# Attention with two feed-forward blocks: the pair's sums in twos behind a slot, one low part put after a slot at the turn, and fewer waits written for TensorE

## The reference

```python
# q, k, v: (2, 8, 768, 64), n_sink 4, window 128
keep = is_sink | in_window
a = softmax(where(keep, scale * q @ k.T, -1e9)); x = a @ v          # (1536, 512)
x = (silu(x @ w_gate) * (x @ w_val)) @ w_out                        # d_ff 1536, stage B
h = x @ w_in; x = (maximum(h, 0) + alpha * minimum(h, 0)) @ w_out2  # d_ff 2048, stage C
```

## Time and profile before

| | |
|---|---|
| time, median of 3 runs | 640.73 us (639.49 to 641.68) |
| the profiled execution's own time | 638.97 us |
| its span | 637.2 us |
| TensorE matmuls busy | 622.4 us, 98% |
| TensorE weight loads busy | 488.4 us, 77% |
| GpSimd busy | 452.2 us, 71% |
| VectorE busy | 407.0 us, 64% |
| ScalarE busy | 243.8 us, 38% |
| granted TensorE clock | full in all 40 slices |

### The profile page before, as it was taken

The page is one execution under the profiler, slowest core; times in us unless marked ns, Lnnn a source line. Parts: engine busy times, 40 slices in busy tenths (PEclk is TensorE's granted clock), DMA queues, the critical chain, the costliest instruction groups (busy, mean ns, idle before and its releaser), DMA issues.

```text
span 637.2 us, 9474 instructions
## 1 busy us (share of the span) xinstructions
PE 622.4 (98%) x3072; PEld 488.4 (77%) x3072; DVE 407.0 (64%) x696; ACT 243.8 (38%) x585; POOL 452.2 (71%) x600
## 2 busy tenths in 40 slices
PE   8889999999998999999999999999999999999998
PEld 5467776777776888888888878887788888888886
DVE  5954667666475866565646474799686567756474
ACT  4735553545534642121212121435544324442150
POOL 6848778878784798999989764779999887810000
PEclk9999999999999999999999999999999999999999
DMA  9343423311321110112212222100222222000004
GB/s 299 110 150 107 136 95 112 117 51 58 97 92 37 33 34 33 67 61 72 68 33 67 89 77 66 33 19 16 67 67 66 67 66 84 17 0 1 1 15 183
DMA packets 29391, 45.67 MB, mean 72 GB/s; under 512 B 2880, under 2 KB 9024, under 8 KB 29344
## 3 DMA queue, kind: packets, MB, share of 16 engines
q1 hardware_dynamic: 29200, 44.81, 21.6%
q10 hardware_dynamic: 144, 0.26, 0.1%
HBM read 41.92 MB, written 3.15 MB: 71 GB/s over the span
## 4 chain that ended last, share of the span: by engine, by line
PE 79%; POOL 9%; DVE 5%; issue 4%; ACT 2%; DMA 1%; SPq 0%; POOLq 0%; DVEq 0%; ACTq 0%
PE ffn_ps L1972 25%; PE att_ps L1946 23%; PE ffn_ps L1887 10%; PE att_ps L1972 7%; PE ffn_ps L1946 6%; POOL w_lo L1657 2%; PE att_ps L1834 2%; POOL scratch L1737 1%; DVE scratch L2199 1%; DMA raw_weights<-pieces 1%; POOL w_hi L1656 1%; PE att_ps L1979 1%; POOL w_lo L1685 1%; PE att_ps L1796 1%; PE att_ps L1887 1%
## 5 line engine op out<-in xcount | busy, mean ns | idle before, releaser
L1657 POOL TENSOR_TENSOR w_lo<-raw_weights,w_hi 128x512 fp32r<-128x512 f32 (+1 forms) x128 | 154.7, 1208 | 10.2
L1656 POOL CAST w_hi<-raw_weights 128x512 fp32r<-128x512 f32 (+1 forms) x128 | 78.5, 613 | 32.5 <-PE ffn_ps L1972 15.8
L2316 DVE TENSOR_TENSOR scratch<-ffn_ps,scratch 128x512 f32<-128x512 f32 x108 | 74.1, 687 | 35.0 <-PE ffn_ps L1972 34.2
L1685 POOL TENSOR_TENSOR w_lo<-part_sum,w_hi 128x256 fp32r<-128x256 f32 x80 | 61.5, 768 | 6.4
L1887 PE MATMUL ffn_ps<-x_hi,w_hi 128*128 128x512 f32 x152 | 61.7, 406 | 1.6 <-issue 0.9
L1887 PE MATMUL ffn_ps<-x_hi,w_lo 128*128 128x512 f32 x152 | 59.5, 391 | 0.0
L1887 PE MATMUL ffn_ps<-x_lo,w_hi 128*128 128x512 f32 x152 | 59.2, 389 | 0.0
L1737 POOL TENSOR_TENSOR scratch<-scratch,inv 128x264 f32<-128x264 f32 (+1 forms) x48 | 30.5, 635 | 31.2 <-DVE inv L2188 31.0
L1972 PE MATMUL ffn_ps<-h_hi,w_hi 128*128 128x512 f32 x130 | 51.6, 397 | 0.0
L1972 PE MATMUL ffn_ps<-h_hi,w_lo 128*128 128x512 f32 x130 | 50.7, 390 | 0.0
L1972 PE MATMUL ffn_ps<-h_lo,w_hi 128*128 128x512 f32 x130 | 50.6, 389 | 0.0
(11 more groups left out here) (210 smaller groups left out, 1574.7 us busy)
## 6 DMA issues: line engine op xcount, KB each, us to landing
raw_weights<-pieces SPq DMA_DIRECT2D x122, 256.0 KB, 2.7
k_sb<-kt SPq DMA_DIRECT2D x12, 264.0 KB, 3.4
v_sb<-vt SPq DMA_DIRECT2D x12, 256.0 KB, 2.7
out<-scratch SPq DMA_DIRECT2D x12, 256.0 KB, 2.0
q_sb<-qt SPq DMA_DIRECT2D x11, 256.0 KB, 3.5
scratch<-vs SPq DMA_DIRECT2D x1, 384.0 KB, 5.4
q_sb<-qt ACTq DMA_DIRECT2D x1, 256.0 KB, 2.5
alpha<-alpha_t SPq DMA_DIRECT2D x1, 8.0 KB, 6.5
```

What stands on the lines that cost most here:

```text
L1656: chain(pool.tensor_copy(hi, raw[:, r % n_raw, at]))
L1657: last = pool.tensor_tensor(lo, raw[:, r % n_raw, at], hi.bitcast(F32), ALU.subtract)
L1685: pool.tensor_tensor(lo, s, hi.bitcast(F32), ALU.subtract).then_inc(split_done, 1)
L2316: ins = dve.tensor_tensor(to, back_ps(key), total, ALU.add)
```

## The change

It has four edits. (1) `emit_slot` no longer returns the four `tsum`s with the low part of a tile; they go to a queue `sums_due`, and after each later slot two of them are put into the plan. (2) A slot with a `tsum` right behind it gets one job of weights in place of two. (3) Around the turn: at `turn_at` the last low part (`x2_rest` 3) comes after the slot in place of before it; a tile's `x_rest` whose slot falls in chunks 65 to 71 is held until after the slot of chunk 72; after the turn an `x_rest` comes one chunk earlier. (4) Some of TensorE's waits are no longer written: in `strip` those for weights at three of seven strips (a later job's wait before it covers them), and in `back` four waits become two on the later of each.

```diff
-            sums = [("tsum", ("B", n, (c - quads_t) // 2)) for n in range(4)] if c > quads_t and c % 2 else []
-            return [("x_rest", c)] + sums
+            return [("x_rest", c)]
         return []
+    def sums_of(c):
+        return [("tsum", ("B", n, (c - quads_t) // 2)) for n in range(4)] if c > quads_t and c % 2 else []
...
+    sums_due, held = [], []
     for n, chunk in enumerate(part_one):
...
         if n == turn_at:
-            plan += now + waiting[0]
-            now, waiting[0] = [], []
+            plan += now
+            now, waiting[0] = waiting[0], []
         for item in slots_here:
-            waiting[1] += emit_slot(item)
+            low = emit_slot(item)
+            for _ in range(2):
+                if sums_due:
+                    plan.append(sums_due.pop(0))
+            for what, c in low:
+                sums_due += sums_of(c)
+                (held if turn_at - 6 <= n <= turn_at else waiting[1 if n < turn_at else 0]).extend(low)
+        if n == turn_at + 1:
+            now = now + held
         plan += now
+    waiting[1] += sums_due
     behind += waiting
...
-        for _ in range(1 if n % 2 else 2):
+        for _ in range(1 if n % 2 or plan[slot_plan[n] + 1][0] == "tsum" else 2):
...
-                if kind == "f":
+                if i == 0:
                     pe.wait_ge(split_done, job_no["piece", piece_key(g, n, part, pair[0])])
-                else:
+                elif a_name in ("S2", "S3", "S4"):
                     pe.wait_ge(split_done, job_no["sum", (g, part, 2 * n + at)])
...
-                    for f in range(F):
-                        pe.wait_ge(split_done, job_no["piece", piece_key(g, f, part, t)])
-                        pe.wait_ge(hlo_done, rest_no[g, f, t])
+                    pe.wait_ge(split_done, max(job_no["piece", piece_key(g, f, part, t)] for f in range(F)))
+                    pe.wait_ge(hlo_done, max(rest_no[g, f, t] for f in range(F)))
```

## The result

| | before | after |
|---|---|---|
| median of 6 runs each, us | 640.72 (639.49 to 642.07) | 635.14 (634.59 to 635.72) |
| profiled execution, own time / span, us | 638.97 / 637.2 | 635.58 / 633.9 |
| instructions | 9474 | 9382 |

The ratio is 0.9912, with a 95% interval of 0.9897 to 0.9926: 5.6 us or 0.88% less, where the forecast said 4.2 us, 0.65%. 635.14 lies within the forecast's range. After the change `strip` is L1961, `back` L1986, the turn of a slot L1827, its values L1848, the normalising L1751, the sums L1725, the spread L2213, the front L1901, the last low parts L2351, a tile's low part L2232, and the pieces' cast and subtraction L1670 and L1671.

What follows compares the result with a forecast made beforehand. The prediction took TensorE, with matmuls 98% of the span, as the bound, so only its standing time could shrink: 2.4 + 1.8 + 0 = 4.2 us off 640.73 gives 636.5 us, range 634.8 to 638.6 us.

Steps and rivals of the forecast that it cites:

- the waits are paid for: Rival: in strips TensorE also gains part of 3.1 us from fewer separate waits; gain over 4.7 us, chance 0.12.
- Edits 1 and 2: forecast 2.4 us: Slots 32, 40 and 48: TensorE's three waits for GpSimd's normalising go wholly, 2.2 to 2.4 us, taken as 2.4.
- the price of slot 32's wait: Slot 32: TensorE's 1.07 us wait for GpSimd's normalising costs 1.12 us, by slot lengths against undisturbed slot 33.
- The other two waits: Slots 40 and 48: TensorE's waits for GpSimd's normalising; with slot 32's they make 2.2 us and go too.
- The turn: forecast 1.8 us: Turn of block 0: second half front starts at about 197.5 instead of 199.30, 1.8 us; 0.9 to 1.9 possible.
- The wait of 0.92: Turn of block 0: the stage C front's wait for low part 1, behind tile 10's low part on VectorE, goes.
- the second wait: Slot 52: TensorE's 0.95 us wait for VectorE's spread, which runs behind the last two low parts.
- Edit 4: forecast 0: Strips and backs: separate waits are issued under running matmuls, so fewer gain 0; upper bound 3.1 us.
- The turn didn't move its wait to GpSimd: Rival: at the turn TensorE waits for GpSimd or low part 3 instead; gain 2.4 to 3.7 us, chance 0.17.
- Weights weren't late: Rival: jobs come up to 9 us later and TensorE stands for late weights; 642 us or more, chance 0.03.
- No change: Rival: stalls in slots 32, 40, 48 only change releaser and GpSimd takes the turn's gain; under 1.9 us, chance 0.08.
- nothing is there to give it back to: From slot 53 on: TensorE's few short waits and GpSimd's late jobs move along, so the gain reaches the end.

Runs made afterwards that it cites:

- before_again: The kernel before, unchanged, run for a second profile: 640.02 us, ratio 0.9986.
- waits_only: The kernel before with only TensorE's waits left out in strips and merged in backs: 639.15 us, ratio 0.9995.
- turn_order: The kernel before with only the last low part of block 0 moved behind the slot at the turn: 639.88 us, ratio 0.9993.
- held_only: The kernel before with only tile 10's low part held until behind slot 52 and tile 11's a chunk earlier: 638.42 us, ratio 0.9982.
- turn_only: The kernel before with only the third edit, both its parts (last low part behind the slot, tile's low part held): 638.66 us, ratio 0.9977.
- before_pieces_first: The kernel before with SyncE's loads of weight pieces issued ahead of its loads of values and keys: 638.51 us, ratio 0.9966.
- after_silu_later: The changed kernel with weight loads ahead of values and keys, and the SiLUs of two groups one chunk later: 635.16 us, ratio 0.9933 against before.
- after_old_waits: The changed kernel with before's TensorE waits put back in strips and backs: 634.9 us, ratio 0.9918 against before.
- after_pieces_first: The changed kernel with SyncE's weight loads issued ahead of its loads of values and keys: 634.69 us, ratio 0.9919 against before.
- sums_only: The kernel before with only the sums in twos behind a slot and one job of weights there: 636.44 us, ratio 0.9943.

## Why the prediction was right, and where its sizes were off

The mechanism held, and so did the side and the range. Two terms of the sum were too small. The gain of 5.6 us lies above the forecast's own 3.7 to 4.7, among the gains that the prediction gave to the rival "the waits are paid for" (over 4.7). That rival's mechanism isn't what happened (edit 4, below), so the range was met with sizes that were off.

**Edits 1 and 2: forecast 2.4 us, measured 3.3 in the stretches, 3.6 by the ratio and 3.0 by the medians.** The step that failed is the price of slot 32's wait, 1.12 us. That is what the one profile had. The stretch of slots 32 and 33 over 9.62 is 1.09, 3.51, 1.65, 1.40, 0.86 and 3.43 us in the six kernels that keep the four sums and the late load (before, before_again, waits_only, turn_order, held_only, turn_only): 1.99 in the mean. The other two waits cost 88.03 - 86.72 = 1.31, near the 1.2 taken. That the load is a cause of the size is shown by before_pieces_first, which removes the stretch's excess with the sums as they were, and by the casts' waits for it: 1.17, 2.12, 1.72, 1.48, 0.92 and 1.82 us, in the same order, each followed by a wait of TensorE of 1.07, 1.90, 1.61, 1.38, 0.84 and 1.79. So four sums and two pieces made GpSimd's queue too long to absorb a late load; fewer sums behind it (edit 1, all but 0.17 and 0.28 us), no piece with a late load in that slot (edit 2) or loading in time removes the stall. What varies from run to run in how late the load is, no run settled.

In two of the six the stretch is 1.6 us longer than the wait explains, before_again and turn_only. There TensorE's granted clock fell soon after the wait. The windows of before_again (stretch, length, busy time of PE, PEld, DVE, ACT and POOL, granted clock, share of the DMA engines, GB/s):

```profile
102.00:104.00 2.00, 0.14 (x4) 0.00 (x0) 1.38 (x4) 0.53 (x3) 1.92 (x4) 1.00 0.12 44
104.00:106.00 2.00, 1.96 (x8) 1.69 (x9) 1.52 (x3) 0.69 (x5) 1.92 (x3) 0.79 0.00 0
106.00:108.00 2.00, 2.00 (x6) 1.52 (x5) 1.02 (x2) 0.00 (x0) 1.92 (x3) 0.50 0.00 0
108.00:110.00 2.00, 2.00 (x13) 0.90 (x12) 0.43 (x1) 0.00 (x0) 1.92 (x3) 0.85 0.00 0
```

After standing for 1.90 us and working for 1.1 it ran at the lower level, 1.2 GHz, for some 3.4 us (0.84 + 2 + 0.6, by what each window lacks of 1.00), which costs half of that; matmuls start 0.43 us apart there (106.09, 106.52) and 0.23 elsewhere. In turn_only, after 1.79 us, the windows show the same (0.66, 0.50 and 0.98 from 104 to 110). After the wait of 1.61 in waits_only it did not fall.

The timed executions bear this out. Of those of the six kernels with the stall, 37 of 125 have a mean granted clock of 0.997 or less; of those of the eight without it, 2 of 52, and one of these two is the profiled one of after_silu_later, whose clock fell in the opening, between 10 and 20 us. Of before's own, 19 of 69 have it, and in each group they take 1.3 to 2.0 us more than the others in the mean. So the lower clock adds about 0.5 us to the mean price of the stall, an estimate: 0.3 of the executions times 1.6 us.

**The turn: forecast 1.8 us, measured 1.16 + 1.01 = 2.17.** The step that failed is "it's near the sum of the two waits, 1.87 us". The wait of 0.92 counts from the end of the transposes, and ends are modelled. By starts, the front of after begins 0.19 us behind its last transposes (192.48 to 192.67) with nothing to wait for; before's transposes start at 194.49, so its front could have started at 194.68 and started at 195.84: 1.16. By the same count the second wait is worth 1.01. The steps on VectorE and GpSimd were right in order and near in time: the values start 1.56 us behind the front here, and I had 1.5; I had the second half of the front at 197.5 with the first at 194.93, 2.57 us apart, and it is 2.45.

**Edit 4: forecast 0, measured 0** (0.9995 alone, and 0.9918 against 0.9912 when undone). 92 instructions left TensorE's queue, 395 separate waits to 303. The `back`'s 42 went too, where I had the build merging them already. Strips and backs took 9.68 and 9.52 us as in the earlier trace rows, which the forecast had as the sign for 0:

```profile
247.31 9.68 PE att_ps L1961 x42
258.37 9.52 PE ffn_ps L1986 x42
```

**The rivals.** The turn didn't move its wait to GpSimd: its normalising started at 193.87 and ended at 194.51, 0.31 us before the transposes of 194.82. Weights weren't late: no wait of TensorE for GpSimd's pieces appears in its waits. "No change" expected the next slots to give the gain back; a wait of 0.7 for the exponentials in slot 31 is the only one of this kind, up by 0.4 us.

**The sum again**: 1.99 + 1.31 + 2.17 = 5.5 us against 5.6 measured. Between the two profiles the second half front came 4.18 us earlier, as forecast at 4.2, but by chance: before's profile had the cheap slot 32 (1.09), and after's lost 0.4 in slot 31. The profiled ends are nearer still, 3.3 us, as the rest of after is 437.27 against 436.47. Most of that is a mixing (gate_sb) that is late for the strip at 312.44, in after's timeline; the matmul ahead of it starts at 311.55, so 0.66 us beyond the 0.23 of a step. The prediction had said of this part that "nothing is there to give it back to". The timeline:

```profile
309.01 1.29 POOL L1671 TENSOR_TENSOR w_lo<-raw_weights,w_hi 128x512 fp32r<-128x512 f32 x1
309.14 1.71 DVE L2320 TENSOR_TENSOR h_lo<-value_sb,h_hi 128x512 fp32r<-128x512 f32 x1
310.26 1.07 POOL L1670 CAST w_hi<-raw_weights 128x512 fp32r<-128x512 f32 x1
...
311.60 0.69 DVE L2252 TENSOR_TENSOR gate_sb<-att_ps,gate_sb 128x512 f32<-128x512 f32 x1
...
312.44 0.47 PE L1961 MATMUL att_ps<-t_hi,w_hi 128*128 128x512 f32 x1 [0.49 <-DVE gate_sb L2252]
```

The same strip tells which edit this goes with. It starts late by 0.49 to 0.66 us in all six kernels that hold a tile's low part back at the turn (held_only, turn_only, after, after_old_waits, after_pieces_first, after_silu_later). In the eight without that part of edit 3 it is late by 0.30 or 0.31 us in three (before_again, sums_only, waits_only) and not at all in five. The views of TensorE's waits of turn_only and before_again show it:

```profile
PE att_ps L1950 <- DVE gate_sb L2242: 0.7, 2, 0.5
```

```profile
PE att_ps L1946 <- DVE gate_sb L2238: 0.2, 1, 0.2
```

The rest is 437.04 us in the mean of the six and 436.68 in the mean of the eight. So about 0.4 us of the gain is given back there, and the sum is nearer to 5.1 us; both it and 5.5 lie inside the interval of the measured ratio, 4.7 to 6.6 us. Why an edit at 193 us changes what happens at 310 us, no run shows, and no version of the change without this delay was tried.

## What to carry to other kernels

An engine that serves the critical one in a fixed order needs slack in every slot: four side jobs in one slot and two pieces more made it the last to arrive, and dropping one piece there was enough alone; spreading them was nearly enough (0.17 and 0.28 us of waits were left). Price a stall from more than one execution when what starts it is a transfer, since here the same wait was 0.84 to 1.90 us; and price it by starts of instructions, not by idle time. Look at what stands in front of a load in its issuing queue: here a load that was free to go stood behind one that had to wait.

## What the runs showed of the hardware

- One wait of 1.79 or 1.90 us in a stretch that was otherwise busy was followed by TensorE's lower clock (1.2 GHz) and some 1.6 us more; one of 1.61 us was not. The kernels with that stall show the lower clock in 37 of 125 executions, those without in 2 of 52.
- Waits as instructions of their own cost TensorE's chain nothing that a median of this kernel shows: 92 fewer of them, and runs of 42 matmuls of the same length to 0.01 us.
- A subtraction of VectorE (L2320) with both inputs in SBUF took 1.71 us; one with an input in PSUM took 0.68 (L2351 above). In the timeline at 309 us, it started at 309.14 beside GpSimd's low part and ended at 310.85, 0.55 us behind that one's end (309.01 + 1.29 = 310.30). GpSimd's cast behind it, 0.61 us elsewhere, took 1.07 and ended 0.48 us behind VectorE. So each ran when the other was through. The Trainium skill ("SBUF — State Buffer", SBUF: two separate sides) says that a VectorE instruction with two SBUF inputs and a GpSimd instruction that reads SBUF share a port pair by an exclusive lock, held for the whole instruction; the trace agrees, by these numbers.
